# Lead expert's hidden layer with the tokens as stationary operand in high and low parts; the next expert's low parts on GpSimd

## The chip, the cores and the metric

One core of one Trainium2 chip. The metric is device time in microseconds of one execution. Engines: TensorE (PE; its weight loads are PEld), VectorE (DVE), ScalarE (ACT), GpSimd (POOL), SyncE (SP, which here only issues DMAs).

## What is computed

Three stages in fp32. First a decayed causal attention without softmax (4 batches, 8 heads, 576 positions, 64 per head), whose result is 2304 tokens of 512. Then a dense mixture of 8 experts, weighted by a matrix that is normalised over rows and columns eight times. Last a mixture in which each token goes to one expert only:

```python
def _moe2_ref(x, w_gate, w1, w2):
    logits = x @ w_gate                       # x [2304, 512], w_gate [512, 8]
    expert_idx = np.argmax(logits, axis=1)
    ...
    for e in range(E):
        mask = expert_idx == e
        xe = x[mask]
        h = np.maximum(xe @ w1[e], 0.0)       # w1[e] [512, 1024]
        ye = h @ w2[e]                        # w2[e] [1024, 512]
        out[mask] = gate_w[mask, None] * ye
```

The change lies in this last stage.

## The kernel before

All blocks of code run side by side, one per engine, and wait for each other on semaphores by count. Names: P = 128, D = 512, F = 1024, ND = D / P = 4, F // P = 8, NT = 18 tiles of tokens, E = 8 experts.

**The order of tiles.** The tokens are scattered in DRAM (`sorted_rows`) so that each expert's lie together, and are worked off in tiles of 128 rows. The expert with most tokens in the first part of the routing, the "lead", comes first (p = 0), so its first two tiles, 0 and 1, can begin before all tokens are routed; they stand as straight code. All other tiles are in loops, `for p in range(E)` with `Fori(start, end)` inside, whose bounds VectorE works out from the counts. Each engine has the same loops (ScalarE L856, VectorE L1299, TensorE L1611; GpSimd has one loop over all tiles from 2 on).

**A tile on TensorE.** `hidden2` (L1563) works out the hidden layer with the weights `Wa` stationary in fp32 and the transposed tokens `x2T` moving: 8 blocks of 128 hidden columns, 4 chunks each, 32 fp32 matmuls of 128 columns, which leave 64 records. The result is already transposed, in banks 0 and 2 (`HB`), four blocks in each. `sorted_T` (L1523) then transposes the next tile's rows (`cur`) into bank 6 (`TB`). `output2` (L1572) works out 8 blocks of three fp32r matmuls of 512 columns: high part times high part (L1577), high times low (L1578), low times high (L1579), into bank 3.

**High and low parts.** A number is split into a high part in fp32r (ScalarE) and the rest (VectorE or GpSimd), and a product is three fp32r matmuls. For the hidden, ScalarE makes `hH` with the relu (`relu2_hi`, L839) and VectorE `hL` (`relu2_lo`). For the second weights of an expert, ScalarE makes `WbH` (`split_w2_hi`, L744) and `WbL` comes from GpSimd for p = 0 (L638) and from VectorE for all others (`split_w2_lo`, L1283).

**VectorE in a tile** (`tile`, L1286), in this order: `move_tile` copies the loaded rows `nxt` to `cur` (L1081); `relu2_lo` twice; `evac_x2T` copies bank 6 to `x2T` (L1085); `result` scales bank 3 to `y` (L1103) and copies `meta` (L1102); `hold` copies the two last columns of `cur` (L1098).

**GpSimd** (`send_tile(done)`, L650): waits until tile `done` is in `cur`, issues the load of tile done + 1 (L648), waits for the result of tile done - 1, and scatters it to `out` (L656). It stands once as straight code, `send_tile(1)`, and then in the loop.

**SyncE** loads `Wa` and `Wb` of the experts three sets deep; the set of p = 3 goes into the place of p = 0 and waits until TensorE has done with the lead's last tile.

## Time and profile before

| | us |
|---|---|
| median of 3 runs | 1925.79 |
| lowest and highest | 1921.24, 1929.61 |
| the profiled execution | 1926.63 |
| its span, first to last instruction | 1925.0 |
| busy TensorE | 1900.1 (99%) |
| busy VectorE | 1131.0 (59%) |
| busy ScalarE | 633.8 (33%) |
| busy GpSimd | 1086.3 (56%) |
| granted TensorE clock, mean | 0.997 |

The last stage begins where TensorE's first matmul of L1567 stands, at 1606.6 us of the span, beside the end of the stage before; from 1638.01 on it is alone, with 22 tiles in all (0 to 21). In the profile a line stands for a group of instructions: its busy time, the mean of one, and what ended the idle time in front of them. Matmuls overlap, so the pitch from start to start, not the length of a record, is what one costs in a row.

### The profile page before, as it was taken

The numbers are of one execution on the slowest core, as the hardware profiler recorded it, in microseconds if no ns is written. First come the engines' busy times: TensorE is split into PE (matmuls) and PEld (weight loads), VectorE is DVE, ScalarE is ACT, GpSimd is POOL, SyncE is SP. The second block draws the span as 40 slices with busy tenths as digits, with TensorE's granted clock in tenths as the row PEclk, the third lists the DMA queues.
The fourth block names the chain that finished last, engine by engine and source line by source line (L and its number), as shares of the span: only waits on it lengthen the run. The fifth ranks groups of instructions, "written<-read, shape, count | busy, mean of one in ns | idle before, by whom it ended". The sixth has DMA issues, their size and how long they took to land.

```text
span 1925.0 us, 32021 instructions
## 1 busy us (share of the span) xinstructions
PE 1900.1 (99%) x11262; PEld 1719.9 (89%) x11262; DVE 1131.0 (59%) x1987; ACT 633.8 (33%) x1107; POOL 1086.3 (56%) x908
## 2 busy tenths in 40 slices
PE   8999999999999999999999999999999999999997
PEld 7889989999998999999999899999999999999997
DVE  4787666566566656555555757555565665322534
ACT  2543343333334333333333433333333332101221
POOL 5766666666587666666667857666666663111111
PEclk9999999999999999999999999999999999999999
DMA  9724444454542222222122222222332223401752
GB/s 229 184 95 148 154 155 152 151 172 159 162 164 69 89 64 78 65 65 65 65 65 66 65 83 88 66 65 65 98 109 95 62 67 115 142 33 57 269 177 71
DMA packets 123356, 209.22 MB, mean 109 GB/s; under 512 B 8910, under 2 KB 58062, under 8 KB 123280
## 3 DMA queue, kind: packets, MB, share of 16 engines
q1 hardware_dynamic: 118240, 192.68, 31.9%
q0 software_dynamic: 5040, 15.51, 2.4%
q8 instruction: 49, 0.80, 0.2%
q14 instruction: 27, 0.22, 0.0%
HBM read 160.03 MB, written 49.19 MB: 109 GB/s over the span
## 4 chain that ended last, share of the span: by engine, by line
PE 95%; DVE 2%; DMA 1%; issue 1%; SPq 0%; ACT 0%; POOL 0%; POOLq 0%; DVEq 0%; ACTq 0%
PE bank L1413 13%; PE bank L1414 13%; PE bank L1415 13%; PE bank L1390 12%; PE bank L1394 12%; PE bank L1392 12%; PE bank L1567 8%; PE bank L1578 2%; PE bank L1577 2%; PE bank L1579 2%; DMA wgraw<-in_moe_w_gate 1%; PE bank L1499 1%; PE bank L1316 1%; PE bank L1347 1%; PE bank L1342 1%
## 5 line engine op out<-in xcount | busy, mean ns | idle before, releaser
L1155 DVE SCALAR_TENSOR_TENSOR acc<-bank,Pw,acc 128x512 f32<-128x512 f32 x516 | 386.5, 751 | 243.4 <-PE bank L1415 231.9
L1415 PE MATMUL bank<-W2H,HL 128*128 128x512 f32 x1152 | 450.3, 391 | 0.0
L1414 PE MATMUL bank<-W2L,HH 128*128 128x512 f32 x1152 | 450.2, 391 | 0.0
L1413 PE MATMUL bank<-W2H,HH 128*128 128x512 f32 x1152 | 450.1, 391 | 0.0
L532 POOL TENSOR_TENSOR W1L<-w1raw,W1H 128x512 fp32r<-128x512 f32 (+1 forms) x190 | 193.8, 1042 | 347.2 <-ACT W1H L692 347.2
L1390 PE MATMUL bank<-XHa,W1H 128*128 128x384 f32 x960 | 323.3, 337 | 2.7 <-ACT Xf L680 0.8
L1394 PE MATMUL bank<-XHa,W1L 128*128 128x384 f32 x960 | 321.1, 335 | 0.0
L1392 PE MATMUL bank<-XLa,W1H 128*128 128x384 f32 x960 | 321.0, 334 | 0.0
L715 ACT ACTIVATE HH<-c 128x384 fp32r<-128x384 f32 x288 | 150.5, 525 | 496.2 <-PE bank L1415 330.2
L1415 PEld LDWEIGHTS bank<-W2H,HL 128*128 128x128 f32 x1152 | 216.2, 188 | 45.3
L1414 PEld LDWEIGHTS bank<-W2L,HH 128*128 128x128 f32 x1152 | 216.3, 188 | 42.5
L1413 PEld LDWEIGHTS bank<-W2H,HH 128*128 128x128 f32 x1152 | 216.4, 188 | 42.2
L537 POOL TENSOR_TENSOR W2L<-w2raw,W2H 128x1024 fp32r<-128x1024 f32 x96 | 230.3, 2399 | 26.9 <-ACT W2H L696 26.9
L532 POOL TENSOR_TENSOR W1L<-Sf,W1H 128x1024 fp32r<-128x1024 f32 x94 | 225.5, 2399 | 0.0
L525 POOL TENSOR_TENSOR Sf<-w1raw 128x256 f32<-128x256 f32 x192 | 148.5, 774 | 136.3 <-DMA w1raw<-in_moe_w 131.1
L715 ACT ACTIVATE HH<-bank 128x384 fp32r<-128x384 f32 x96 | 47.1, 491 | 456.4 <-PE bank L1415 456.4
L1390 PEld LDWEIGHTS bank<-XHa,W1H 128*128 128x128 f32 x960 | 180.2, 188 | 5.6 <-issue 2.4
L1133 DVE SCALAR_TENSOR_TENSOR HL<-c,HH 128x384 fp32r<-128x384 f32 x288 | 175.2, 612 | 11.5
L1392 PEld LDWEIGHTS bank<-XLa,W1H 128*128 128x128 f32 x960 | 180.3, 188 | 0.0
L1394 PEld LDWEIGHTS bank<-XHa,W1L 128*128 128x128 f32 x960 | 180.2, 188 | 0.0
L1117 DVE TENSOR_TENSOR c<-cs,bank 128x384 f32<-128x384 f32 x96 | 53.1, 553 | 204.0 <-PE bank L1394 204.0
L1567 PEld LDWEIGHTS bank<-x2T,Wa 128*128 128x128 f32 x1408 | 160.9, 192 | 1.9
(192 smaller groups left out, 2684.2 us busy)
## 6 DMA issues: line engine op xcount, KB each, us to landing
w1raw<-in_moe_w SPq DMA_DIRECT2D x96, 512.0 KB, 3.5
w2raw<-in_moe_w SPq DMA_DIRECT2D x96, 512.0 KB, 3.7
sorted_rows<-blank SPq DMA_DIRECT2D x147, 257.0 KB, 3.6
Wa<-in_moe_w SPq DMA_DIRECT2D x7, 2048.0 KB, 7.9
Wb<-in_moe_w SPq DMA_DIRECT2D x7, 2048.0 KB, 9.3
QK<-qk SPq DMA_DIRECT2D x24, 384.0 KB, 10.3
KV<-kv SPq DMA_DIRECT2D x24, 384.0 KB, 11.7
nxt<-sorted_rows POOLq DMA_DIRECT2D x23, 257.0 KB, 2.9
```

The source lines that it names most:

```text
L532: nc.gpsimd.tensor_tensor(W1L[s][:, blk, :], raw, W1H[s][:, blk, :].bitcast(F32), ALU.subtract).then_inc(s_w1l, 1)
L537: nc.gpsimd.tensor_tensor(W2L[s][:, :, :], w2raw[:, :, :], W2H[s][:, :, :].bitcast(F32), ALU.subtract).then_inc(s_w2l, 1)
L715: nc.scalar.activation(HH[:, i, :], source, ACT.Relu).then_inc(s_hhi, 1)
L1133: nc.vector.scalar_tensor_tensor(HL[:, i, :], source, 0.0, HH[:, i, :].bitcast(F32), ALU.max, ALU.subtract).then_inc(s_hlo, 1)
L1155: ins = nc.vector.scalar_tensor_tensor(tile, psum, weight, tile, ALU.mult, ALU.add)
L1390: mm(bank[b][:, 0:W], W1H[s][:, blk, :], XH[i][:, c, :], start=start and c == 0, stop=False, skip_group_check=True)
L1392: mm(bank[b][:, 0:W], W1H[s][:, blk, :], XL[i][:, c, :], start=False, stop=False, skip_group_check=True)
L1394: last = mm(bank[b][:, 0:W], W1L[s][:, blk, :], XH[i][:, c, :], start=False, stop=(c == NK - 1), skip_group_check=True)
L1413: mm(dst, HH[:, h, tok], W2H[s][:, m, :], start=(m == 0), stop=False)
L1414: mm(dst, HH[:, h, tok], W2L[s][:, m, :], start=False, stop=False)
L1415: last = mm(dst, HL[:, h, tok], W2H[s][:, m, :], start=False, stop=(m == 1))
L1567: last = mm(bank[HB[j // 4]][:, (j % 4) * P:(j % 4 + 1) * P], Wa[s][:, a, j * P:(j + 1) * P], x2T[:, a, :], start=(a == 0), stop=(a == ND ...
```

## The change

Of the lead's tiles, those in the loop (tile 2 and on) get another hidden layer. The tokens are split into `xH` (ScalarE, from bank 6) and `xL` (VectorE), and stand in the array; the lead's first weights are split once, `WaH` (ScalarE, four pieces of 128x1024) and `WaL` (VectorE, in the place of `Wa[0]`), and move, 512 columns at a time. A half (512 hidden columns) is 12 fp32r matmuls. Its result is not transposed: ScalarE's relu writes it to `hs` in SBUF, TensorE transposes it in four blocks into bank 4 or 5 (`HT`), and from there ScalarE and VectorE make `hH` and `hL`. On TensorE the next tile's `sorted_T` stands between the quarters of the second half, and the second half's transposes behind the first block of the output layer.

The low parts of the second weights of p = 1 go from VectorE to GpSimd, which does them behind `send_tile(2)`, now straight code; its loop begins at 3. On VectorE the tokens' low parts and `x2T` of tile 2 stand in front of the low parts of the lead's matrix, and those in front of the result of tile 1. Tiles 0 and 1 and all other experts' tiles keep their code.

```diff
--- before.py
+++ after.py
@@ -298,6 +298,16 @@
         for s in range(3):
             WbH.append([place(f"WbH{s}_{j}", [P, D], F32R, at)[0] for j, at in enumerate(ats[s])])
 
+
+        at_lead = at_t + WB
+        WaH = [place(f"WaH{j}", [P, F], F32R, at)[0]
+               for j, at in enumerate([at_lead + j * 4 * F for j in range(ND - 1)] + [at_rows])]
+        WaL, _ = place("WaL0", [P, ND, F], F32R, at_rows + RSTEP)
+        hs, a = place("hs", [P, F], F32, at_rows + 4 * F)
+        xH, a = place("xH", [P, ND, P], F32R, a)
+        xL, a = place("xL", [P, ND, P], F32R, a)
+        assert a <= at_rows + RSTEP and at_lead + (ND - 1) * 4 * F <= at_small
+
         sorted_rows = nc.dram_tensor("sorted_rows", [FILL * (E - 1) * P, ROW], F32, kind="Internal").ap()
 
         bank = [ctx.enter_context(nc.psum_tensor(f"bank{i}", [P, 512], F32)) for i in range(8)]
@@ -332,6 +342,7 @@
         s_xs, s_T, s_x2T, s_cur, s_meta = sem("s_xs"), sem("s_T"), sem("s_x2T"), sem("s_cur"), sem("s_meta")
         s_g1, s_hi2, s_lo2, s_y, s_yev, s_out = sem("s_g1"), sem("s_hi2"), sem("s_lo2"), sem("s_y"), sem("s_yev"), sem("s_out")
         s_held = sem("s_held")
+        s_wah, s_wal, s_xh2, s_hr, s_ht = (sem(f"s_{x}") for x in ("wah", "wal", "xh2", "hr", "ht"))
 
         block = ctx.enter_context(nc.Block())
 
@@ -351,6 +362,7 @@
 
         HB = (0, 2)
         YB = 3
+        HT = (4, 5)
 
         w1v = w11.rearrange("e (a p) (q f) -> e q p a f", p=P, q=NQ)
         w2v = w12.rearrange("e (q a p) d -> e q p a d", p=P, q=NQ)
@@ -658,8 +670,14 @@
                     in_=y[:, :], in_offset=None, bounds_check=last_row, oob_is_err=False).then_inc(s_out, 16)
 
             send_tile(1)
+            send_tile(2)
+            pool.wait_ge(s_wal, ND)
+            for j in range(F // P):
+                pool.wait_ge(s_w2hi, F // P + j + 1)
+                nc.gpsimd.tensor_tensor(WbL[1][:, j, :], Wb[1][:, j, :], WbH[1][j][:, :].bitcast(F32),
+                                        ALU.subtract).then_inc(s_w2lo, 1)
             total = pool.value_load(bounds[0:1, E:E + 1], min_val=E, max_val=MAXT)
-            with pool.Fori(2, total + 1) as done:
+            with pool.Fori(3, total + 1) as done:
                 send_tile(done)
             pool.wait_ge(s_xs, total * 16 + 16)
             pool.wait_ge(s_out, total * 16)
@@ -850,14 +868,47 @@
             relu2_hi(0, (0,))
             routing_exp(NG - 1)
             relu2_hi(0, (1,))
-            relu2_hi(1, (0, 1))
+
+            def lead_w1_hi(a):
+                nc.scalar.activation(WaH[a][:, :], Wa[0][:, a, :], ACT.Copy).then_inc(s_wah, 1)
+
+            def tokens_hi(n):
+
+                act.wait_ge(s_T, n + 1)
+                nc.scalar.activation(xH[:, :, :], bank[TB][:, :].rearrange("p (a i) -> p a i", a=ND),
+                                     ACT.Copy).then_inc(s_xh2, 1)
+
+            def lead_relu(i, g):
+                act.wait_ge(s_g1, i * 2 + g + 1)
+                nc.scalar.activation(hs[:, g * 4 * P:(g + 1) * 4 * P], bank[HB[g]][:, :], ACT.Relu).then_inc(s_hr, 1)
+
+            def lead_hi(i, g):
+                act.wait_ge(s_ht, i * 2 + g + 1)
+                nc.scalar.activation(hH[:, 4 * g:4 * g + 4, :], bank[HT[g]][:, :].rearrange("p (a i) -> p a i", a=4),
+                                     ACT.Copy).then_inc(s_hi2, 1)
+
+            act.wait_ge(s_l2, TS * K)
+            for a in range(ND - 1):
+                lead_w1_hi(a)
+            relu2_hi(1, (0,))
+            act.wait_ge(s_scat, 16 * NT)
+            lead_w1_hi(ND - 1)
+            relu2_hi(1, (1,))
+            tokens_hi(2)
             split_w2_hi(1)
             act.wait_ge(s_bounds, 1)
             for p in range(E):
                 start = act.value_load(bounds[0:1, p:p + 1], min_val=2, max_val=MAXT)
                 end = act.value_load(bounds[0:1, p + 1:p + 2], min_val=2, max_val=MAXT)
                 with act.Fori(start, end) as i:
-                    relu2_hi(i, (0, 1))
+                    if p == 0:
+                        lead_relu(i, 0)
+                        lead_hi(i, 0)
+                        lead_relu(i, 1)
+                        tokens_hi(i + 1)
+                        lead_hi(i, 1)
+                    else:
+                        relu2_hi(i, (0, 1))
                 if p + 2 < E:
                     split_w2_hi(p + 2)
 
@@ -1278,29 +1329,69 @@
 
             def split_w2_lo(p):
 
+                dve.wait_ge(s_w2lo, p * (F // P))
                 for j in range(F // P):
                     dve.wait_ge(s_w2hi, p * (F // P) + j + 1)
                     nc.vector.tensor_tensor(WbL[p % 3][:, j, :], Wb[p % 3][:, j, :], WbH[p % 3][j][:, :].bitcast(F32),
                                             ALU.subtract).then_inc(s_w2lo, 1)
+
+            def tokens_lo(n):
+
+                dve.wait_ge(s_xh2, n - 1)
+                nc.vector.tensor_tensor(xL[:, :, :], bank[TB][:, :].rearrange("p (a i) -> p a i", a=ND),
+                                        xH[:, :, :].bitcast(F32), ALU.subtract)
+
+            def lead_lo(i, g):
+                dve.wait_ge(s_hi2, i * 2 + g + 1)
+                h = slice(4 * g, 4 * g + 4)
+                nc.vector.tensor_tensor(hL[:, h, :], bank[HT[g]][:, :].rearrange("p (a i) -> p a i", a=4),
+                                        hH[:, h, :].bitcast(F32), ALU.subtract).then_inc(s_lo2, 1)
+
+            def send(i):
+                dve.wait_ge(s_out, i * 16)
+                result(i)
+                dve.wait_ge(s_meta, i + 1)
+                dve.wait_ge(s_yev, i + 1)
+                hold(i + 1)
 
             def tile(i):
                 dve.wait_ge(s_held, i + 1)
                 move_tile(i + 1)
                 relu2_lo(i, (0, 1))
                 evac_x2T(i + 1)
-                dve.wait_ge(s_out, i * 16)
-                result(i)
-                dve.wait_ge(s_meta, i + 1)
-                dve.wait_ge(s_yev, i + 1)
-                hold(i + 1)
-
-            tile(1)
-            split_w2_lo(1)
+                send(i)
+
+            def lead_tile(i):
+                dve.wait_ge(s_held, i + 1)
+                move_tile(i + 1)
+                lead_lo(i, 0)
+                tokens_lo(i + 1)
+                evac_x2T(i + 1)
+                lead_lo(i, 1)
+                send(i)
+
+
+            nc.vector.memset(lg[0:1, 0, 0:1], 0.0).then_inc(s_hr, 4)
+            nc.vector.memset(lg[0:1, 0, 1:2], 0.0).then_inc(s_ht, 4)
+            dve.wait_ge(s_held, 2)
+            move_tile(2)
+            relu2_lo(1, (0, 1))
+            tokens_lo(2)
+            evac_x2T(2)
+            dve.wait_ge(s_g1, 4)
+            for a in range(ND):
+                dve.wait_ge(s_wah, a + 1)
+                nc.vector.tensor_tensor(WaL[:, a, :], Wa[0][:, a, :], WaH[a][:, :].bitcast(F32),
+                                        ALU.subtract).then_inc(s_wal, 1)
+            send(1)
             for p in range(E):
                 start = dve.value_load(bounds[0:1, p:p + 1], min_val=2, max_val=MAXT)
                 end = dve.value_load(bounds[0:1, p + 1:p + 2], min_val=2, max_val=MAXT)
                 with dve.Fori(start, end) as i:
-                    tile(i)
+                    if p == 0:
+                        lead_tile(i)
+                    else:
+                        tile(i)
                 if p + 2 < E:
                     split_w2_lo(p + 2)
 
@@ -1569,15 +1660,35 @@
                     if j % 4 == 3:
                         last.then_inc(s_g1, 1)
 
-            def output2(i, p, s):
-                for j in range(F // P):
+            def lead_hidden(i, g, chunks):
+
+                cols = slice(g * 4 * P, (g + 1) * 4 * P)
+                for a in chunks:
+                    mm(bank[HB[g]][:, :], xH[:, a, :], WaH[a][:, cols], start=(a == 0), stop=False)
+                    mm(bank[HB[g]][:, :], xL[:, a, :], WaH[a][:, cols], start=False, stop=False)
+                    if g == 0:
+                        pe.wait_ge(s_wal, a + 1)
+                    last = mm(bank[HB[g]][:, :], xH[:, a, :], WaL[:, a, cols], start=False, stop=(a == ND - 1))
+                if chunks[-1] == ND - 1:
+                    last.then_inc(s_g1, 1)
+
+            def lead_T(i, g):
+                pe.wait_ge(s_hr, i * 2 + g + 1)
+                for j in range(4):
+                    last = nc.tensor.transpose(bank[HT[g]][:, j * P:(j + 1) * P],
+                                               hs[:, (4 * g + j) * P:(4 * g + j + 1) * P], ident)
+                last.then_inc(s_ht, 1)
+
+            def output2(i, p, s, blocks=range(F // P)):
+                for j in blocks:
                     if j % 4 == 0:
                         pe.wait_ge(s_w2lo, p * (F // P) + j + 4)
                         pe.wait_ge(s_lo2, i * 2 + j // 4 + 1)
                     mm(bank[YB][:, :], hH[:, j, :], WbH[s][j][:, :], start=(j == 0), stop=False)
                     mm(bank[YB][:, :], hH[:, j, :], WbL[s][:, j, :], start=False, stop=False)
                     last = mm(bank[YB][:, :], hL[:, j, :], WbH[s][j][:, :], start=False, stop=(j == F // P - 1))
-                last.then_inc(s_y, 1)
+                if blocks[-1] == F // P - 1:
+                    last.then_inc(s_y, 1)
 
             pe.wait_ge(s_hlo, 4 * K - 3)
             pe.wait_ge(s_w2[0], weights_landed(0))
@@ -1611,6 +1722,19 @@
             for p in range(E):
                 start = pe.value_load(bounds[0:1, p:p + 1], min_val=2, max_val=MAXT)
                 end = pe.value_load(bounds[0:1, p + 1:p + 2], min_val=2, max_val=MAXT)
+                if p == 0:
+                    with pe.Fori(start, end) as i:
+                        pe.wait_ge(s_x2T, i + 1)
+                        lead_hidden(i, 0, range(ND))
+                        lead_hidden(i, 1, range(ND // 2))
+                        lead_T(i, 0)
+                        sorted_T(i + 1)
+                        lead_hidden(i, 1, range(ND // 2, ND))
+                        pe.wait_ge(s_held, i + 1)
+                        output2(i, 0, 0, (0,))
+                        lead_T(i, 1)
+                        output2(i, 0, 0, range(1, F // P))
+                    continue
                 with pe.Fori(start, end) as i:
                     pe.wait_ge(s_w2[p % 3], weights_landed(p))
                     hidden2(i, p % 3)
```

## Rows read from the trace of the kernel before

**Rows 1.** The page: busy time by engine, and the chain that ended last.

```profile
PE 1900.1 (99%) x11262; PEld 1719.9 (89%) x11262; DVE 1131.0 (59%) x1987; ACT 633.8 (33%) x1107; POOL 1086.3 (56%) x908
...
PE 95%; DVE 2%; DMA 1%; issue 1%; SPq 0%; ACT 0%; POOL 0%; POOLq 0%; DVEq 0%; ACTq 0%
```

**Rows 2.** The chain in order of time, last stage: start us, us, what.

```profile
1638.01 7.14 PE bank L1567 x64
1645.16 0.44 PE bank L1526 x4
1645.59 0.24 PE bank L1577
...
1651.20 7.14 PE bank L1567 x64
...
1769.88 7.14 PE bank L1567 x64
```

**Rows 3.** Timeline of ScalarE: start us, us, instructions, idle before and its releaser.

```profile
1645.19 0.60 ACT L842 ACTIVATE hH<-bank 128x512 fp32r<-128x512 f32 x1 [2.98 <-PE bank L1567]
1645.69 4.26 ACT L747 ACTIVATE WbH<-Wb 128x512 fp32r<-128x512 f32 x8
...
1777.06 0.60 ACT L842 ACTIVATE hH<-bank 128x512 fp32r<-128x512 f32 x1 [2.98 <-PE bank L1567]
1777.55 4.26 ACT L747 ACTIVATE WbH<-Wb 128x512 fp32r<-128x512 f32 x8
```

**Rows 4.** Timeline of TensorE: four transposes between two groups of output matmuls.

```profile
1611.99 0.39 PE L1415 MATMUL bank<-W2H,HL 128*128 128x512 f32 x1
1612.23 0.60 PE L1488 MATMUL bank<-ktab,acc 128*128 128x128 f32 x4
1612.58 0.48 PE L1413 MATMUL bank<-W2H,HH 128*128 128x512 f32 x1
1612.89 0.40 PE L1414 MATMUL bank<-W2L,HH 128*128 128x512 f32 x1
```

**Rows 5.** Groups by line, last stage: busy us, mean ns | idle before.

```profile
L1526 PE MATMUL bank<-ktab,cur 128*128 128x128 f32 x92 | 13.8, 273 | 0.0
L1526 PEld LDWEIGHTS bank<-ktab,cur 128*128 128x128 f32 x92 | 10.9, 142 | 0.1
```

**Rows 6.** Timeline of VectorE around tiles 1 and 2.

```profile
1645.82 0.69 DVE L1091 SCALAR_TENSOR_TENSOR hL<-bank,hH 128x512 fp32r<-128x512 f32 x1 [2.31 <-ACT hH L842]
...
1651.30 0.17 DVE L1102 COPY meta<-held 128x2 f32<-128x2 f32 x1 [4.19 <-PE bank L1579]
1651.38 0.74 DVE L1103 TENSOR_SCALAR y<-bank,held 128x512 f32<-128x512 f32 x1
...
1652.29 4.89 DVE L1283 TENSOR_TENSOR WbL<-Wb,WbH 128x512 fp32r<-128x512 f32 x8
```

**Rows 7.** Single lines of VectorE: ns min/median/max, first and last start us.

```profile
L963 DVE TENSOR_TENSOR W1L<-Sf,W1H x2: 1210/2172/3135, 96.4 to 105.8; 128x1024 fp32r<-128x1024 f32 x2
...
L1081 DVE COPY cur<-nxt x23: 417/430/1111, 1555.0 to 1904.8; 128x514 f32<-128x514 f32 x23
```

**Rows 8.** GpSimd: timeline, its splitting line, and the page's DMA issue.

```profile
1639.48 0.57 POOL L648 DMA_DIRECT2D nxt<-sorted_rows  x1 [3.53 <-DVE y L1103]
...
1644.25 0.57 POOL L648 DMA_DIRECT2D nxt<-sorted_rows  x1 [2.88 <-issue]
1652.94 1.53 POOL L656 DMA_INDIRECT out<-y,meta  x1 [8.12 <-DVE y L1103]
...
1666.11 1.10 POOL L656 DMA_INDIRECT out<-y,meta  x1 [6.67 <-DVE y L1103]
1667.68 0.57 POOL L648 DMA_DIRECT2D nxt<-sorted_rows  x1 [0.47 <-issue]
...
L638 POOL TENSOR_TENSOR WbL<-Wb,WbH x8: 1281/1296/1474, 1596.5 to 1605.4; 128x512 fp32r<-128x512 f32 x8
...
nxt<-sorted_rows POOLq DMA_DIRECT2D x23, 257.0 KB, 2.9
```

## The prediction

> **What bounds the kernel now.** I read the page's first and fourth parts first [rows 1]: TensorE is busy for 99% of the span and 95% of the chain that ended last is its own work. So the time changes only by what the change adds to or takes from TensorE's stream, or by a wait that it puts there. Next I read the chain in order of time through the last stage [rows 2]. A tile there is three pieces without a gap: the hidden layer (L1567, 7.14 us), four transposes of the next tile's tokens (L1526, 0.44 us), and the output layer (24 matmuls, from 1645.59 to 1651.20, 5.61 us). That is 13.19 us. ScalarE's rows say how many tiles the change touches [rows 3]: the split for the third expert, which stands behind the lead's loop, starts at 1777.55, just after the relu (1777.06) of the tile whose hidden layer starts at 1769.88. From 1651.20, where tile 2 starts, to 1769.88 are nine tiles of 13.19 us. So the loop of p = 0 runs over tiles 2 to 11, ten tiles; tiles 0 and 1 and the ten behind tile 11 keep their code.
>
> **TensorE's work in a lead tile.** Removed: the 7.14 us of L1567. Added: 24 matmuls of 512 columns (two halves, four chunks, three products). They have the shape and type of the output layer's 24, so by that row 5.61 us. Also added: eight transposes. The four of L1488 between two output groups [rows 4] take, start of the last matmul before to start of the second behind, 1612.89 - 1611.99 = 0.90 us, of which two matmul pitches are 0.47; so four transposes are 0.43 to 0.44, and eight are 0.88. Gross gain: 7.14 - 5.61 - 0.88 = 0.65 us a tile, 6.5 us in ten. The two outer bounds of the pitch: between outputs earlier it is 0.23 (the same rows), which would give 0.1 us a tile more, 1 us in all; nothing in the rows gives a longer one. The records of a transpose last 273 ns each [rows 5], since they overlap; if in the new place they ran one after the other, eight would be 2.18 us.
>
> The Trainium skill ("TensorE: Matmul & The Clock Gate", Part 4) gives about 275 ns for a 128x128 transpose in a kernel. Taken as a cost in the stream, that speaks against this change; the record's length agrees with it and the stream's pitch does not, so I let the pitch decide. The rule's outcome is the third rival.
>
> **New hand-overs in a lead tile.** Time t runs from the tile's start; m is 0.234.
> - First half. Its 12 matmuls end at 2.81. ScalarE starts a relu 0.03 to 0.10 behind the matmul's end and takes 0.60 [rows 2, 3, 6], so it is done by 3.5. TensorE fills the time with six matmuls (to 4.21): hidden. Its transposes are done at 4.65, ScalarE's high part at 5.3, VectorE's low part (0.69 [rows 6]) at 6.0. TensorE does the next tile's transposes (5.09) and six matmuls (6.49) and needs it at 6.3, one weight load ahead: hidden, by 0.3.
> - Second half. Its matmuls end at 6.49, the relu runs from 6.58 to 7.18, and the one output block in front of the transposes ends at 7.19. The transposes' weights are the relu's result, so their load (0.14 [rows 5]) and a hand-over (0.05; ScalarE to VectorE shows 0.03 [rows 3, 6]) are bare: 0.2 us lost a tile. I take **0.22**. Between zero, if the end of a matmul is seen early, and 0.6, if each of the three hand-overs costs 0.1 more.
> - Low part of the second half. The transposes end at 7.85. ScalarE has put the next tokens' high part in between (starts follow each other by 0.50 [rows 3]), and takes the second high part from 7.9 to 8.5. VectorE does the tokens' low part from 7.7, the copy to x2T from 8.3 and the low part of the hidden from 8.93 to 9.62 (pitch 0.61, 4.89 / 8 [rows 6]). Blocks 1 to 3 keep TensorE until 9.95, and it needs the weights at 9.76. Cover 0.1 us, so I count nothing; if each VectorE operation costs 0.1 more, 0.2 us a tile is lost.
>
> The tile is then 13.19 - 0.65 + 0.22 = 12.76 us, and ten of them bring **-4.3 us**. The end of the tile is as before: result, hold and the copy of the next rows (L1102, L1103, L1098, L1081) start 0.1 us behind the last matmul, and no one waits for them until the transposes at 4.65.
>
> **The entrance: the lead's matrix.** ScalarE makes three high parts once it is done with tile 0's relu (from about 1632.7, 1.05 to 1.07 us each, twice the step of 4.26 / 8 of its 512 pieces [rows 3]) and the fourth behind tile 1's first relu. It was idle there; its waits for the scatters of the routed rows are met, since GpSimd's load at 1639.48 stood behind the same count. Then come tile 1's second relu at 1645.19, the tokens' high part at 1645.7, and the split of the next expert 0.5 us later than before, which nobody waits for until tile 12. VectorE: low part of tile 1's hidden at 1645.82, tokens' low part 1646.43, copy 1647.04, and then four low parts of 128x1024. The least of L963's two is 1.21 us, the other 3.14, where GpSimd worked beside it [rows 7]; here GpSimd has only the load at 1644.25, so I take 1.15 to 1.2 as the step: 1647.7 to 1652.3. TensorE needs the first at 1651.6 and the fourth at 1653.7: covered by 1.4 us. At 3.14 us each they would end at 1660.2 and cost 6.5 us. Behind them on VectorE stands the result of tile 1: 1653.0 in place of 1652.12 [rows 6].
>
> **GpSimd: the split that goes there.** This is the wait that I do count. Eight low parts of 128x512 at 1.28 to 1.30 us [rows 8] are 10.2 us; on VectorE they took 4.89 us under cover [rows 6]. In front of them stand the load of tile 3 (still at 1644.25) and the sending of tile 1, which needs that result: y is seen 0.8 us later (1652.12 to 1652.94), so it starts at 1653.8 and takes 1.1 (at 1652.94 it took 1.53) [rows 8]. The split runs from about 1655.2 to 1665.4. Queued behind it is the load of tile 4, which before waited for nothing but VectorE's copy of tile 3. Between a send's end (1667.21) and the next load's start are 0.47 us; with the registers of the loop's entrance I take 1.0, bounds 0.4 and 2.5. Load at 1666.4, landed 2.9 later [rows 8], copied to cur in 0.43 [rows 7]: 1669.8, with hand-over and weight load 1670.0. TensorE wants it in tile 3 at 1663.96 + 4.65 = 1668.6. **+1.5 us**, once; the bounds are 0 and 3. From tile 4 on GpSimd is back in step (load 5 waits only for the copy of tile 4, at 1671), and the sends need only 2.8 us of each 12.8.
>
> **Moved with it at no cost.** The loads of expert 3 hang on the end of the lead's last tile, so they move along with what waits for them. GpSimd's eight low parts are done 100 us before tile 12 needs them. The extra wait of VectorE's split for the third expert is on that same count. The two memsets are some 0.1 us on an idle engine.
>
> **Sum.** -6.5 + 2.2 + 1.5 = -2.8 us. The profiled execution was 1926.63 us with a span of 1925.0; it lies 0.8 above the median of 1925.79, so I subtract from the median: **1923.0 us**.
>
> **Rivals.**
> 1. *The entrance is fully covered.* The span's numbers of GpSimd are rough; if the split ends 1.5 us earlier, no stall is left: -4.3 us, 1921.5. For it: TensorE's need comes late in tile 3. Against it: every row of L638 is 1.28 or more. With the short pitch too, 1920.
> 2. *The second half's chain is late in every tile.* Seven operations on ScalarE and VectorE stand between the last hidden matmul and block 4, with 0.1 us of cover. With 0.3 us lost at the transposes and 0.3 to 0.6 at block 4, ten tiles give back 6 to 9 us of 6.5: with the entrance +1 to +4, 1927 to 1930. For it: all covers are thin, and a hand-over into TensorE is hardly shown. Against it: the same engines' pitches are constant to 0.01 us in the rows.
> 3. *Transposes cost their records' length* in the new places: 8 x (0.273 - 0.109) = 1.31 us a tile, 13.1 in all: -2.8 + 13.1 = +10.3, 1936. Against it: three groups of four between matmuls of this very shape at 0.44.
> 4. *VectorE and GpSimd get into each other's way* (the one that ends slower by a single place). VectorE's operations from SBUF alone have been stretched beside GpSimd: L963 from 1.21 to 3.14, L1081 from 0.43 to 1.11 [rows 7]. If the lead's low parts or the split are stretched, the load of tile 4 comes later one for one. It decides once that load is 4.3 us behind its need, that is 2.8 us later than I have it: pieces of 1.65 us in place of 1.29 are enough. At 2.0 us a piece: 5.7 more, +2.9, 1928.7.
>
> The Trainium skill ("SBUF — State Buffer") calls that pair of ports an exclusive lock between a VectorE operation with two inputs in SBUF and a GpSimd one that reads SBUF. By that rule the four low parts here find GpSimd free, and in the split's 10 us VectorE's work has one input in PSUM, so both rows should come out unstretched; the stretched rows of [rows 7] agree, where both engines read SBUF.
>
> **Chances.** Forecast case 0.60 (1921.5 to 1925); rival 1 0.12; rival 2 0.16; rival 4 0.09; rival 3 0.03. The range takes the first four nearly whole: 1918.5 to 1929.5. About 0.5%, 9.6 us, is what a measurement of this kernel can tell from no change. The gross gain of 6.5 us plus 1 is under that, so faster has 0.03; slower has rival 3 and the ends of 2 and 4, 0.06; the rest, 0.91, is within.
>
> **What would show it.** Right: the lead's tiles start every 12.7 to 12.8 us, and TensorE has a gap of 0.2 us in front of the second four transposes and of about 1.5 us in tile 3 before the transposes of cur. L1283's first eight are gone from VectorE, and L638 has sixteen. Wrong: a gap in front of output block 4, a gap behind the wait for the matrix' low parts in tile 2, lead tiles of 13.2 us or more, or a number of lead tiles other than ten.

## The result, and the profile after

| | before | after |
|---|---|---|
| median, us | 1925.32 | 1932.01 |
| lowest to highest of 20 runs | 1919.28 to 1931.23 | 1928.93 to 1936.5 |
| after to before | | 1.0032 (1.0022 to 1.0042) |
| the profiled execution, its span | 1926.63, 1925.0 | 1929.93, 1927.9 |

The change makes the kernel 0.32% slower, some 6.2 us by the ratio. I had forecast 2.8 us faster, 1923.0, with a range of 1918.5 to 1929.5. The time lies outside that range and on the other side of before. It is within the 0.5% that I had called no change, but that bound was too wide: the ratio is known to 0.1%, and no change lies outside its interval.

Profiled executions differ by some microseconds in where tile 1 begins (1628.7 to 1639.7 us in the runs here), though the change has hardly touched the code in front of it. So I measure the stage that the change touches by its own rows: from the start of the transposes behind tile 1's hidden layer to the start of the same transposes in tile 12, the first tile of the next expert. In the profile before this is 1790.05 - 1644.99 = 145.06 us, after it is 1792.99 - 1641.41 = 151.58 us: **+6.5 us**, the whole difference. "Stage" below is this length, less 145.06.

The waits of TensorE in the last stage, after: who waited for whom, us in total, times, longest.

```profile
PE bank L1617 <- DVE cur L1132: 9.1, 1, 9.1
PE bank L1607 <- DVE pos L1080: 0.2, 1, 0.2
```

The first row was not there before. L1617 is the transposes of the next tile's rows, L1132 the copy of these rows to `cur`. The timelines of VectorE and GpSimd in that place, in tile 2, answer to [rows 6] and [rows 8]:

```profile
1648.65 0.74 DVE L1154 TENSOR_SCALAR y<-bank,held 128x512 f32<-128x512 f32 x1
1649.48 0.17 DVE L1149 COPY held<-cur 128x2 f32<-128x2 f32 x1
1651.33 9.99 DVE L1132 COPY cur<-nxt 128x514 f32<-128x514 f32 x1 [1.67 <-issue]
1661.24 0.68 DVE L1347 TENSOR_TENSOR hL<-bank,hH 128x512 fp32r<-128x512 f32 x1
...
1650.21 1.01 POOL L668 DMA_INDIRECT out<-y,meta  x1 [8.10 <-DVE y L1154]
1651.21 9.81 POOL L677 TENSOR_TENSOR WbL<-Wb,WbH 128x512 fp32r<-128x512 f32 x8
1662.67 0.58 POOL L660 DMA_DIRECT2D nxt<-sorted_rows  x1 [1.64 <-issue]
```

GpSimd's eight pieces begin at 1651.21. VectorE's copy, 0.43 us by its median [rows 7], begins 0.12 us later and lasts 9.99 us. It is done 0.3 us behind the last piece. What that does to TensorE, in its timeline and in the table by stretch (the number behind POOL's count is the granted clock):

```profile
1651.63 0.60 PE L1678 MATMUL bank<-ktab,hs 128*128 128x128 f32 x4
1661.37 1.11 PE L1617 MATMUL bank<-ktab,cur 128*128 128x128 f32 x4 [9.14 <-DVE cur L1132]
1662.14 0.78 PE L1667 MATMUL bank<-WaH,xH 128*128 128x512 f32 x1
1662.71 0.63 PE L1668 MATMUL bank<-WaH,xL 128*128 128x512 f32 x1
1663.14 0.63 PE L1671 MATMUL bank<-WaL,xH 128*128 128x512 f32 x1
...
1660.00:1665.00 5.00, 3.63 (x11) 3.05 (x12) 1.92 (x2) 0.00 (x0) 1.60 (x2) 0.50 0.18 51
1665.00:1670.00 5.00, 5.00 (x21) 4.01 (x20) 1.98 (x3) 1.68 (x3) 0.00 (x0) 0.80 0.00 2
```

TensorE stands for 9.1 us. Its clock is granted at 1.00 up to 1656, falls to 0.50, the 1.2 GHz level, before 1657, while TensorE stands, and is back at 1.00 from about 1667. Until then its matmuls follow each other every 0.43 us and not every 0.23. From 1661.37 to the same transposes of tile 3 at 1676.50 are 15.13 us, where an undisturbed tile has 12.66: 2.5 us more. A tile in the steady part of the lead's loop, after:

```profile
1676.07 0.60 PE L1678 MATMUL bank<-ktab,hs 128*128 128x128 f32 x4
1676.50 0.60 PE L1617 MATMUL bank<-ktab,cur 128*128 128x128 f32 x4
...
1678.79 0.39 PE L1689 MATMUL bank<-WbH,hL 128*128 128x512 f32 x1
1679.17 0.66 PE L1678 MATMUL bank<-ktab,hs 128*128 128x128 f32 x4
...
1689.15 0.60 PE L1617 MATMUL bank<-ktab,cur 128*128 128x128 f32 x4
...
1701.82 0.60 PE L1617 MATMUL bank<-ktab,cur 128*128 128x128 f32 x4
```

The lead's tiles come every 12.66 us (1676.50, 1689.15, 1701.82), where they came every 13.19 [rows 2]. The only gap is in front of the second half's transposes, 1679.17 - 1678.79 - 0.23 = 0.15 us.

So the account of the stage is 10 x (12.66 - 13.19) = -5.3, +9.1 idle, +2.5 low clock: +6.3 of the +6.5 measured. The gain in the lead's tiles is there. A single meeting of two engines takes it back and more.

### The profile page after: what moved, and what is told of

It is laid out like the page before. It is cut to its first block and busy times, and to the rows that moved or that the text cites. A ratio compares the mean times of both kernels' runs of the same rounds, so it can differ in the third digit from the quotient of the medians.

```text
span 1927.9 us, 31447 instructions
## 1 busy us (share of the span) xinstructions
PE 1898.6 (98%) x10942; PEld 1702.9 (88%) x10942; DVE 1147.4 (60%) x1996; ACT 655.5 (34%) x1142; POOL 1096.0 (57%) x916
## 5 line engine op out<-in xcount | busy, mean ns | idle before, releaser
L1184 DVE SCALAR_TENSOR_TENSOR HL<-c,HH 128x384 fp32r<-128x384 f32 x288 | 175.5, 613 | 11.4
L668 POOL DMA_INDIRECT out<-y,meta x22 | 23.4, 1063 | 195.2 <-DVE y L1154 194.9
```

The source lines that it names most:

```text
L1184: nc.vector.scalar_tensor_tensor(HL[:, i, :], source, 0.0, HH[:, i, :].bitcast(F32), ALU.max, ALU.subtract).then_inc(s_hlo, 1)
```

## The experiments

**First question: is the meeting the cause?** Theory A says yes; B says that the copy is late for a reason of its own; C says that the new tiles cost.

`e1_split_behind_copy`, GpSimd:

```diff
             pool.wait_ge(s_wal, ND)
+            pool.wait_ge(s_cur, 4)
             for j in range(F // P):
```

> The changed kernel with one wait more: GpSimd's eight low parts begin only when VectorE has copied tile 3's rows to cur. Theory A (the copy of tile 3's rows in tile 2, 9.99 us in the changed kernel, was held up by GpSimd's eight pieces, which had begun 0.12 us earlier): the copy takes 0.43 us, TensorE's 9.1 us of idle time and its slow stretch behind it are gone; the load of tile 4 then goes out behind the split, at about 15.5 us from tile 2's start, and costs 1 to 1.5 us in tile 3. Lead tiles stay at 12.66 us, so -5.3 + 1.5 = -3.8 against the kernel before, 1921.5. Theory B (the copy is late for another reason, its rows or its own queue): it stays at 8 to 10 us and the time at 1932. Theory C (the lead's tiles are what costs): the copy gets short and the time stays above the kernel before's.

Measured: ratio 0.9964 (0.9947 to 0.9981), median 1919.57, stage -4.5.

```profile
1651.41 0.43 DVE L1133 COPY cur<-nxt 128x514 f32<-128x514 f32 x1 [1.68 <-issue]
...
1660.47 0.32 DVE L1154 COPY meta<-held 128x2 f32<-128x2 f32 x1 [3.28 <-PE bank L1690]
...
1651.99 10.02 POOL L678 TENSOR_TENSOR WbL<-Wb,WbH 128x512 fp32r<-128x512 f32 x8 [0.68 <-issue]
1661.95 0.58 POOL L660 DMA_DIRECT2D nxt<-sorted_rows  x1
```

With the copy first it takes 0.43 us, and the kernel is faster than before. TensorE waits only 0.5 us, in tile 3, since the load of tile 4 goes out right at the split's end and not 1.0 us behind it, as I had it. A holds. B and C fall.

`e2_split_tile_later`, GpSimd:

```diff
             send_tile(2)
+            send_tile(3)
             pool.wait_ge(s_wal, ND)
...
-            with pool.Fori(3, total + 1) as done:
+            with pool.Fori(4, total + 1) as done:
```

> The changed kernel with the split one more tile load and send later on GpSimd (behind the load of tile 4 and the sending of tile 2). Theory A: the split begins about 1 us behind the copy of tile 4's rows and ends before tile 4 wants tile 5's rows, so neither the copy nor a load is late: ten tiles at 12.66 us in place of 13.19, -5.3 us, 1920.0. Theory B: a copy of 8 to 10 us is there again, in whichever tile. Theory C: above 1925.

Measured: 0.9949 (0.9931 to 0.9967), median 1919.18, stage -5.2. TensorE does not wait anywhere from tile 1 on. The copy of tile 4's rows (1667.29) is 1.3 us ahead of the split (1668.60), which follows the indirect DMA at once as in the changed kernel; no other copy asks before its last piece. This kernel is faster than the kernel before and the changed one, by the stage 0.7 us ahead of e1; the intervals of the two overlap.

`e3_split_on_vector` puts the part back: no straight `send_tile(2)` and no split on GpSimd (its loop begins at 2 again), and on VectorE, without the wait in front that the change had added to `split_w2_lo`,

```diff
             send(1)
+            split_w2_lo(1)
             for p in range(E):
```

> The changed kernel with p = 1's low parts back on VectorE, behind the result of tile 1, as in the kernel before; the lead's tiles as changed. Theory A: no work of GpSimd holds the copy, but the 4.9 us of low parts stand in front of it: it starts about 7.1 us from tile 2's start where TensorE wants its result at 4.7: 2.9 us of idle time in tile 2, none in tile 3. -5.3 + 2.9 = -2.4, 1922.9. Theory B: as the changed kernel. Theory C: slower than before by 2 or more.

Measured: 0.999 (0.9973 to 1.0008), median 1924.19, stage -2.4, TensorE 2.6 us idle before the same transposes (cur is copied at 1651.73, 6.9 us from tile 2's start). By the stage that is A's number. The interval alone does not tell it from before. So there is a reason to move the split: left on VectorE it costs half of the gain.

`e4_only_split_moved` is the kernel before with the lines below, and with GpSimd's loop and VectorE's wait as in the changed kernel:

```diff
             send_tile(1)
+            send_tile(2)
+            for j in range(F // P):
+                pool.wait_ge(s_w2hi, F // P + j + 1)
+                nc.gpsimd.tensor_tensor(WbL[1][:, j, :], Wb[1][:, j, :], WbH[1][j][:, :].bitcast(F32),
+                                        ALU.subtract).then_inc(s_w2lo, 1)
...
             tile(1)
-            split_w2_lo(1)
```

> The kernel before with one part of the change alone: p = 1's low parts on GpSimd behind the load of tile 3 and the sending of tile 1, everything else as before. Theory A: the copy of tile 3's rows meets the split here too and ends with it, some 13 us from tile 2's start, where TensorE wants it at 7.14: 5.5 to 6 us idle, and 0 to 2 us for a lower clock behind it: +6 to +8, 1932. If the copy happens to be first, +0 to +1. Theory B or C (the cause lies in the new tiles or in the new operations on VectorE): within 1 us of the kernel before.

Measured: 1.0045 (1.0027 to 1.0062), median 1934.0, stage +7.7.

```profile
1651.90 10.00 DVE L1086 COPY cur<-nxt 128x514 f32<-128x514 f32 x1 [1.68 <-issue]
...
1651.79 9.82 POOL L664 TENSOR_TENSOR WbL<-Wb,WbH 128x512 fp32r<-128x512 f32 x8
...
PE bank L1531 <- DVE cur L1086: 5.8, 1, 5.8
```

The same hold, with none of the new tiles or operations. TensorE wants the rows later in an old tile, so it stands for 5.8 us. The clock is at 0.50 here too, from about 1659, while TensorE stands, to about 1665.

**Second question: why eight pieces?** A request that waits for the piece under way would have cost 1.2 us. I had such a case: the copy of 1.11 us [rows 7], at 1601.94, in the fifth of eight pieces, was let in at that piece's end. The same copy takes 1.09 to 1.12 us in the same place in every kernel here but e8. From the timelines of the kernel before:

```profile
1594.10 2.40 POOL L537 TENSOR_TENSOR W2L<-w2raw,W2H 128x1024 fp32r<-128x1024 f32 x1 [8.98 <-ACT W2H L696]
1596.46 10.24 POOL L638 TENSOR_TENSOR WbL<-Wb,WbH 128x512 fp32r<-128x512 f32 x8
...
1601.94 1.11 DVE L1081 COPY cur<-nxt 128x514 f32<-128x514 f32 x1
```

It is not alone. In that profile 70 of VectorE's operations without an operand in PSUM take at least 0.15 us more than the shortest of their line and form; none of them spans a whole GpSimd operation that began more than 0.06 us behind its own start. One conversion of three columns, 0.17 us alone, shows it best. GpSimd's next operation stood right behind the one that it met:

```profile
654.26 2.40 POOL L537 TENSOR_TENSOR W2L<-w2raw,W2H 128x1024 fp32r<-128x1024 f32 x1 [0.20 <-ACT W2H L696]
656.62 2.40 POOL L532 TENSOR_TENSOR W1L<-Sf,W1H 128x1024 fp32r<-128x1024 f32 x1
...
654.35 2.33 DVE L1048 CAST sloti<-slot 128x3 uint32<-128x3 f32 x1
```

So a hold over several pieces is the exception in these traces. The next runs change when and how the copy asks.

`e5_gap_between_pieces`, GpSimd: each piece waits for the one before it to be written.

```diff
                 pool.wait_ge(s_w2hi, F // P + j + 1)
+                pool.wait_ge(s_w2lo, F // P + j)
```

> The changed kernel, in which GpSimd waits before each of the eight pieces until its own piece before has been written, so that no two pieces follow each other at once. Theory L (the line: VectorE's copy gets the port only where GpSimd leaves a gap between two operations): the copy of tile 3's rows takes 1.6 us or less, one piece and itself, TensorE waits 0.5 us or less in tile 2, and the load of tile 4, which goes out behind the split at 13 to 14 us of tile 2, costs 1 us: 1921 to 1922. Theory S (once started, GpSimd keeps the port until it has nothing more to do with it): the copy still takes 9 to 10 us, the time is 1932.

Measured: 0.9997 (0.9978 to 1.0016), median 1922.3, stage -3.1. The copy takes 1.50 us. TensorE waits 1.6 us in all, 0.65 in tile 2 and the rest in tile 3: the eight pieces now last 11.38 us, and the load of tile 4 is later. L holds, S falls.

`e6_copy_in_first_piece` puts one operation from the output bank to `hL` (0.69 us) in front of `hold(2)` on VectorE; `e7_copy_in_later_piece` three of them.

> The changed kernel with one operation more on VectorE (a copy of the output bank into a tile that is overwritten, some 0.8 us) in front of hold(2). The copy of tile 3's rows then asks 0.8 to 0.9 us behind the begin of the first piece, not 0.12. Theory S or L, with any piece: it is released with the last piece, 9.1 us long, 1932. Theory N (only a request in the first tenths of a microsecond loses; later in a piece it gets in at the piece's end, as the copy of 1.11 us did in the kernel before): 0.8 to 1.2 us long, TensorE waits 0.6 us in tile 2, and 1921 to 1922.

> As the one before with three such operations in a row, so that the copy of tile 3's rows asks some 2.4 to 2.9 us behind the begin of the split, in its second or third piece. Theory S or L: released with the last piece at the same moment as in the changed kernel, 7 to 7.5 us long, 1932. Theory N: one piece at most, so 0.5 to 1.7 us long, done at about 7 us of tile 2 where TensorE wants it at 4.7: 2.5 us idle and no slow clock, 1922 to 1923.

Measured: e6 1.0052 (1.002 to 1.0083), stage +5.5; the copy asks 0.86 us behind the split's begin and takes 9.25. e7 1.0056 (1.0021 to 1.0091), stage +6.9; here it was `hold`'s copy of two columns that asked, 0.46 us behind the begin, and it took 9.38. So e7 did not test a later piece; it showed that a copy of two columns is held as well as one of 514. N falls for the first piece.

`e8_copy_as_reduce`, VectorE:

```diff
-                nc.vector.tensor_copy(cur[:, :], nxt[:, :]).then_inc(s_cur, 1)
+                nc.vector.tensor_reduce(cur[:, D + 1:ROW].bitcast(I32), nxt[:, D + 1:ROW].bitcast(I32).unsqueeze(2), AX.X, ALU.max)
+                nc.vector.tensor_reduce(cur[:, 0:D + 1], nxt[:, 0:D + 1].unsqueeze(2), AX.X, ALU.max).then_inc(s_cur, 1)
```

> The changed kernel, in which VectorE moves the rows to cur with a maximum over an axis of length one (a reduction, one of 513 and one of 1 column) and not with a copy; it meets GpSimd's split at the same moment. Theory F (it is the form of the operation, a copy from SBUF to SBUF, that needs what GpSimd holds): the reduction takes 0.7 us, TensorE does not wait in tile 2, and the time is 1920 to 1922. If any operation of VectorE that reads SBUF is held: 9 to 10 us, 1932.

Measured: 0.998 (0.9963 to 0.9996), median 1921.66, stage -4.9.

```profile
1654.38 0.68 DVE L1133 TENSOR_REDUCE cur<-nxt 128x513 f32<-128x513 f32 x1
...
1654.20 10.00 POOL L677 TENSOR_TENSOR WbL<-Wb,WbH 128x512 fp32r<-128x512 f32 x8
```

The reduction starts 0.18 us behind the first piece and is not held at all, though the split follows the indirect DMA as before. It is the form of the operation. The reduction is no free remedy: it replaces the copy in every tile, and of the nine steps from tile to tile behind tile 12 six are 13.34 to 13.36 us long, where before none is over 13.19. The runs do not show why.

`e9_copy_in_second_piece` and `e10_copy_in_fourth_piece` put two and six operations behind `hold(2)`, each from an idle PSUM bank, so that nothing asks before the copy:

```diff
             send(1)
+            for _ in range(2):
+                link(nc.vector.tensor_scalar(hL[:, 0:4, :], bank[7][:, :].rearrange("p (a i) -> p a i", a=4), 1.0,
+                                             None, ALU.mult))
```

> The changed kernel with two filler operations on VectorE (each from an idle PSUM bank, some 0.75 us) behind hold(2), so that the copy of tile 3's rows asks 1.5 to 1.7 us behind the split's begin, in the second of the eight pieces, with nothing of VectorE having asked in the first. If any request during the line of pieces is held to its end: the copy takes about 8 us and ends at the split's end, 1932. If only a request in the first piece is held so: 1.3 us at most, TensorE waits about 2 us in tile 2, no slow clock, 1922 to 1923.

> As the one before with six fillers: the copy asks 4.4 to 5 us behind the split's begin, in the fourth or fifth piece, where the copy of the kernel before got in at the piece's end. Held to the end: about 5.3 us long and 1932. Held for one piece: 1.6 us at most, done at 9 to 9.7 us of tile 2 where TensorE wants it at 4.7, so 4.5 to 5 us idle, clock perhaps lower for a few us behind it: 1924 to 1927.

Measured: e9 1.0037 (1.0014 to 1.006), stage +5.6; e10 1.0029 (1.0014 to 1.0043), stage +6.3. The copies ask 1.94 and 4.52 us behind the begin, in the second and the fourth piece, and take 8.17 and 5.59 us: both to the end of the eight.

`e11_split_in_two_fours` puts `send_tile(3)` between the fourth and the fifth piece (GpSimd's loop then begins at 4).

> The changed kernel with the split cut in two: four pieces where the eight were, then the load of tile 4 and the sending of tile 2, then the other four. If the copy is held as long as pieces stand in line, the hold scales with their number: released after four, about 5.1 us long (4 x 1.226 - 0.12 + 0.43) and not 9.99; TensorE waits 4.2 us in tile 2, the clock perhaps falls for a shorter time, the load of tile 4 is in time: -5.3 + 4.2 + 0 to 1.5, so 1924 to 1926. If the hold is a fixed time or ends with something else: 10 us and 1932.

Measured: 1.001 (0.9996 to 1.0025), median 1926.35, stage +0.6. TensorE waits 4.3 us.

```profile
1650.27 5.14 DVE L1134 COPY cur<-nxt 128x514 f32<-128x514 f32 x1 [1.67 <-issue]
...
1650.15 4.96 POOL L679 TENSOR_TENSOR WbL<-Wb,WbH 128x512 fp32r<-128x512 f32 x4
```

Four pieces last 4.96 us and the copy beside them 5.14. The hold scales with the number of pieces in line. The clock is at 1.00 through the 4.3 us, and at 0.50 from about 1656.2 to 1659.5, when TensorE works again; the tile is 1.4 us longer for it (14.09 us to the next tile's transposes, for 12.66).

**Third question: why were two copies let in?** `e12_probes_split_after_wait` lets GpSimd wait in front of the split for the landing of tile 1's rows, and puts probes on VectorE:

```diff
             pool.wait_ge(s_wal, ND)
+            pool.wait_ge(s_out, 32)
...
             send(1)
+            idle = bank[7][:, :].rearrange("p (a i) -> p a i", a=4)
+            for kind in "ffffffpffpffp":
+                if kind == "f":
+                    link(nc.vector.tensor_scalar(hL[:, 0:4, :], idle, 1.0, None, ALU.mult))
+                else:
+                    link(nc.vector.tensor_copy(lg[:, 0, 0:2], lg[:, 1, 0:2]))
```

`e13_probes` has the probes alone; `e14_probes_fillers_read_sbuf` has fillers that also read a table in SBUF.

> The changed kernel with probes on VectorE behind the result of tile 1: six operations from an idle PSUM bank, a copy of two columns from SBUF to SBUF, two operations, a copy, two operations, a copy; and GpSimd waits, before the split, until tile 1's rows have landed in out, so that the split does not follow the indirect DMA at once and begins some 2.8 us later, at about 5.6 us of tile 2. Hypothesis D (the port is kept through the whole line only where the pieces stood in line behind the indirect DMA): each probe copy that asks during the split takes at most 1.4 us, and the time is 1925 to 1928 for the fillers. Otherwise the first that asks is held to the split's end, 7 us or more, and the time is 1931 to 1935.

> The same probes without that wait: the split begins as in the changed kernel, and the first probe copy asks about 2.9 us behind its begin, in the third piece. By what the copies that asked in the first, second and fourth piece showed it is held to the end, about 7 us, 1931 to 1935. If it is let in at the piece's end (1.4 us at most), requests differ by their size or by chance.

> As e13_probes, but each filler reads a table in SBUF beside the PSUM bank, as VectorE's low parts of the hidden do. Hypothesis E (an operation of VectorE that reads SBUF while the line runs leaves the port open for the next request; the two copies that got in at a piece's end, in the kernel before and in e1_split_behind_copy, had such operations in front of them, the held ones had not): the first probe copy takes at most 1.4 us, and the time is 1925 to 1928. Otherwise about 7 us and 1931 to 1935, as e13_probes.

Single times: 1922.99, 1938.55 and 1936.65 beside 1926.02 for the kernel before; stages +5.2 (the fillers), +11.0 and +11.4. What counts is the probes. First of e12, then of e13:

```profile
1651.64 0.96 DVE L1394 COPY lg<-lg 128x2 f32<-128x2 f32 x1
1654.45 0.84 DVE L1133 COPY cur<-nxt 128x514 f32<-128x514 f32 x1 [1.86 <-issue]
...
1644.62 1.01 POOL L668 DMA_INDIRECT out<-y,meta  x1 [8.77 <-DVE y L1155]
1648.87 10.03 POOL L678 TENSOR_TENSOR WbL<-Wb,WbH 128x512 fp32r<-128x512 f32 x8 [3.24 <-issue]
```

```profile
1658.06 7.16 DVE L1393 COPY lg<-lg 128x2 f32<-128x2 f32 x1
...
1654.37 1.01 POOL L668 DMA_INDIRECT out<-y,meta  x1 [8.83 <-DVE y L1154]
1655.38 9.82 POOL L677 TENSOR_TENSOR WbL<-Wb,WbH 128x512 fp32r<-128x512 f32 x8
```

In e12 the split begins behind a wait, and two copies, in the third and the fifth piece, each get in at that piece's end; a probe near the end of the first piece (1649.97) took 0.18 us. In e13 the split begins 1.01 us behind the begin of the indirect DMA, and the copy in the third piece is held to the end; in e14 likewise, 7.17 us. What D forecast came, and E falls. But e12 changes two things at once: GpSimd really waits, and the split begins 3.24 us behind the indirect DMA's end. These runs do not tell which of the two counts. My times for all three were too low by their stages: I had not counted how long the fillers, and in e13 and e14 the hold, keep the rows from TensorE (8.7 us in e12, 14.5 in e13 and e14).

`e15_small_op_before_split` puts `nc.gpsimd.tensor_tensor(lg[:, 3, :], lg[:, 1, :], lg[:, 2, :], ALU.add)` in front of the split; `e16_one_gap` has

```diff
                 pool.wait_ge(s_w2hi, F // P + j + 1)
+                if j == 1:
+                    pool.wait_ge(s_w2lo, F // P + 1)
```

> The changed kernel with one small GpSimd addition (128x8, about 0.2 us) between the sending of tile 1 and the split, without a wait. If the hold needs the indirect DMA directly in front of the pieces, the copy of tile 3's rows (asked about 0.1 us before or behind the first piece) takes 1.7 us at most and the time is 1920 to 1922. If it needs only that the pieces stand in line without a wait between them and the indirect DMA, the copy takes 9 to 10 us and the time is 1932.

> The changed kernel in which GpSimd waits for its own result once, in front of the second piece, and not before each (e5). The copy asks in the first piece and should get in at that one gap: 1.5 us long, TensorE waits about 0.6 us in tile 2; the split is done at 10.2 us of its begin and the load of tile 4 costs 0.5 to 1 us: 1920.5 to 1922. If every piece needs its own gap, or what lets the copy in is the slower pace and not the gap: 8 to 10 us long, 1932.

Measured: e15 1.0025 (1.0011 to 1.0039), stage +6.2, the copy takes 10.14 us: a small operation in between does not help. e16 0.998 (0.996 to 1.0001), median 1921.58, stage -4.3, the copy takes 1.51 us, TensorE waits 0.7: one gap is enough. Of e16:

```profile
1655.84 1.51 DVE L1134 COPY cur<-nxt 128x514 f32<-128x514 f32 x1 [1.67 <-issue]
...
1655.73 10.26 POOL L679 TENSOR_TENSOR WbL<-Wb,WbH 128x512 fp32r<-128x512 f32 x8
```

The copies from SBUF to SBUF that asked during a line of these pieces while at least one more was to come:

| kernel | asked behind the split's begin, us | took, us | in front of the pieces |
|---|---|---|---|
| after | 0.12 | 9.99 | indirect DMA |
| e4 | 0.11 | 10.00 | indirect DMA |
| e6 | 0.86 | 9.25 | indirect DMA |
| e7 | 0.46 | 9.38 | indirect DMA |
| e9 | 1.94 | 8.17 | indirect DMA |
| e10 | 4.52 | 5.59 | indirect DMA |
| e11 (four pieces) | 0.11 | 5.14 | indirect DMA |
| e13, e14 | 2.68, 2.70 | 7.16, 7.17 | indirect DMA |
| e15 | -0.05 | 10.14 | indirect DMA, small operation |
| before | 5.48 | 1.11 | a wait of 8.98 us, then one operation |
| e1 | 8.48 | 0.32 | a wait |
| e12 | 1.10, 2.77, 5.58 | 0.18, 0.96, 0.84 | a wait |
| e5, e16 | 0.12, 0.11 | 1.50, 1.51 | indirect DMA, then a gap behind the first piece |

Copies that asked in the last piece, or just in front of it (e1, e2, e5, e8, e16), took 0.17 to 0.75 us; they cannot tell a hold for one piece from a hold to the end.

## Why the prediction was wrong

Point by point, by its own steps:

- **TensorE's work, 0.65 us a tile.** Right. The matmuls of the new hidden layer follow each other by 0.23 us, and four transposes take 1676.50 - 1676.07 = 0.43 us. Ten tiles, as worked out. Rival 3 (transposes at 273 ns) is refuted in every tile.
- **Hand-overs, 0.22 us a tile.** The mechanism and the place were right, the size was 0.15, so the tile is 12.66 and not 12.76 us. The chain in front of output block 4 stayed hidden with its 0.1 us of cover. Rival 2 did not happen.
- **The lead's matrix.** Right: four low parts in 4.62 us (I had 4.6), no wait of TensorE for them.
- **The split's own length.** Right within 0.4 us (9.81 to 10.03, against 10.2). It began 3.76 us from tile 2's start, where I had 4.0.
- **The load of tile 4, +1.5 us.** The mechanism was right, the size too large, and it was not what set the time. In e1 it is 0.5 us: the load goes out with no gap behind the split, where I had 1.0. In the changed kernel it is nothing, because tile 3 comes 9 us later.
- **The step that failed** is the sentence on the end of the tile: result, hold and the copy of the next rows "start 0.1 us behind the last matmul, and no one waits for them until the transposes at 4.65". I gave the copy no time of its own. In tile 2 it stands behind the entrance of VectorE's loop and asks 3.88 us from the tile's start (1651.33 - 1647.45), 1.67 us of which the profile calls issue. Before, that was hidden behind VectorE's own 4.89 us of low parts [rows 6]. Taking these away moved the copy into the split. For the split's stretch I then wrote that "VectorE's work has one input in PSUM" and left out the one operation that does not: the copy of the rows. A row that I had shown spoke for it. I said that the stretched rows agree with a lock of operations with two inputs in SBUF, but L1081 has one input there and went from 0.43 to 1.11 us [rows 7].
- **Rival 4** named the two engines, the one-for-one delay and even the stretched copy of 1.11 us, and gave 0.09 to it. But it priced the meeting as pieces that get longer, and the load of tile 4 as the one who waits. The pieces did not get longer at all; the copy waited for all eight. Had I priced one meeting as one piece, by [rows 7], it would have been 1.2 us; the true price was 9.1 us of TensorE's time, and 2.5 more for the clock, which I had nowhere.

The lock that the Trainium skill ("SBUF — State Buffer", Who interferes with whom) describes explains who meets whom: it puts copies among VectorE's operations that can take both ports, and says that a reduction never contends. e8 agrees, with 0.68 us against 9.99. It also says that the one who comes second waits for the other's instruction. e1, e5, e12, e16 and the kernel before agree with that (0.2 to 1.5 us); after, e4, e6, e7, e9 to e11 and e13 to e15 do not: there the copy waited for up to eight instructions, and the measurement decides.

What stays open: why a line of pieces behind the indirect DMA keeps VectorE out while one behind a wait does not. The runs show that a wait behind the first piece is enough to end it (e16), that no hold came where a wait stood in front of the pieces (e1, e12), and that an operation in between does not help (e15). What GpSimd holds meanwhile, no profile here shows. In the kernel before GpSimd had waited 8.98 us one operation ahead of its line, and no indirect DMA is near it. So the table does not part three readings: that the indirect DMA causes the hold, that the missing wait does, or that the short time behind the DMA does. A line behind other work without a wait, in the place of the indirect DMA, was not tried.

## What to carry to other kernels

Before work is moved to GpSimd, list what VectorE does from SBUF to SBUF in the same stretch, with the time at which each of them will ask after the move, and put the small copies that someone waits for in front. If a long line of GpSimd operations must stand near them, place it where no copy asks (e2, stage -5.2), or cut it with one wait on its own result behind the piece that the copy will meet. In e16 that wait made the line 10.26 us long, for 10.02 in e1, and the copy still waited for one piece (stage -4.3). An operation that was hidden behind the work that you take away (here the loop's entrance) starts earlier afterwards: ask what it runs into.

## What the runs showed that I had not expected

- A VectorE copy of two columns, 0.17 us alone, took 7.2 to 9.4 us beside GpSimd operations of 1.23 us each (e7, e13, e14). For the copy of the rows, a single semaphore wait between two of these brought 9.99 us down to 1.51 (e16).
- TensorE's clock stayed at 1.00 through and behind 2.6 us of idle time in e3. In e11 it fell to 0.50 only behind the 4.3 us idle, in e4 and after while TensorE stood (5.8 and 9.1 us). On top of the idle time that cost 1.4 us in e11, 1.8 in e4 and 2.5 after.
